# Four transfers instead of one for y and for x, spread between the loads of a weight ring

## What is computed

```
x  = attention(q, k, v, mem_k, mem_v)            # 3072 x 512, chunks of 32 with a small context
h  = x @ w_in;   g = elu(h);                     y = g @ w_out        # layer one
h2 = y @ w_in2;  g2 = s * relu(h2)**2 + b;       out = g2 @ w_out2    # layer two
```

## Time and profile before

| | |
|---|---|
| time, median of three runs | 1216.26 us (1216.18 to 1216.88) |
| profiled execution | 1211.64 us |
| its span, first to last instruction | 1209.9 us |
| mean granted TensorE clock | 0.975 of full |
| transfers in the span | 302.80 MB, mean 250 GB/s |

### The profile page before, as it was taken

One profiled execution on the slowest core, in us unless ns is written; L12 is line 12 of the kernel. 1 busy time (PEld: TensorE's weight loads), 2 busy tenths in 40 slices (PEclk: granted clock), 3 DMA queues, 4 the chain that ended last, 5 costly groups with the idle time before them and its releaser, 6 DMA issues.

```text
span 1209.9 us, 18083 instructions
## 1 busy us (share of the span) xinstructions
PE 1116.7 (92%) x5787; PEld 880.7 (73%) x5787; DVE 845.4 (70%) x1246; ACT 757.0 (63%) x1775; POOL 425.8 (35%) x458
## 2 busy tenths in 40 slices
PE   8993998988899899989899898899999999999998
PEld 4662776766677778767687676677787887887876
DVE  5773478448966965896848966948938559567385
ACT  4864687567656857747647557657566476566463
POOL 5789369743231322134334265672001010000000
PEclk9986999999999999999999999999999999999999
DMA  9994999999788888859997599887587666786664
GB/s 213 270 270 150 292 334 312 315 306 301 228 280 219 257 248 262 265 188 349 303 288 226 165 352 396 299 311 231 177 233 259 196 193 175 198 225 189 192 189 157
DMA packets 203750, 302.80 MB, mean 250 GB/s; under 512 B 112520, under 2 KB 120712, under 8 KB 203656
## 3 DMA queue, kind: packets, MB, share of 16 engines
q1 hardware_dynamic: 203656, 301.65, 81.8%
HBM read 226.10 MB, written 75.50 MB: 249 GB/s over the span
## 4 chain that ended last, share of the span: by engine, by line
PE 55%; DVE 12%; DMA 6%; issue 5%; ACT 5%; POOL 4%; SPq 0%; ACTq 0%; DVEq 0%; POOLq 0%
PE ps L1004 28%; PE ps L989 23%; DMA w_ring<-w_scratch 3%; DVE g_lo L1442 2%; DVE X L1354 2%; ACT ps L1084 2%; DVE xc_lo L1347 1%; DVE T L1437 1%; DVE X L1437 1%; POOL w_new L774 1%; PE ps L903 1%; DVE X L1411 1%; PE ps L955 1%; POOL att L774 1%; ACT elu L1163 1%
## 5 line engine op out<-in xcount | busy, mean ns | idle before, releaser
L989 PE MATMUL ps<-xc_hi,w_ring 128*128 128x512 f32 x1344 | 438.3, 398 | 24.2 <-issue 9.8
L1004 PE MATMUL ps<-g_hi,w_ring 128*128 128x512 f32 x1344 | 423.6, 396 | 26.9 <-issue 15.9
L989 PEld LDWEIGHTS ps<-xc_hi,w_ring 128*128 128x128 f32 x1344 | 254.9, 190 | 84.0 <-issue 13.6
L1004 PEld LDWEIGHTS ps<-g_hi,w_ring 128*128 128x128 f32 x1344 | 248.2, 189 | 92.6 <-issue 28.2
L989 PE MATMUL ps<-xc_lo,w_ring 128*128 128x512 f32 x672 | 263.9, 393 | 0.0
L1004 PE MATMUL ps<-g_lo,w_ring 128*128 128x512 f32 x672 | 263.3, 392 | 0.0
L774 POOL TENSOR_TENSOR w_new<-w_raw,w_new 128x256 fp32r<-128x256 f32 x182 | 167.0, 921 | 207.6 <-ACT w_new L1216 204.2
L1442 DVE TENSOR_TENSOR g_lo<-X,g_hi 128x512 fp32r<-128x512 f32 x240 | 187.9, 789 | 45.5 <-ACT g_hi L1202 45.0
L1202 ACT ACTIVATE g_hi<-X 128x512 fp32r<-128x512 f32 x240 | 149.2, 628 | 80.2 <-PE ps L1004 76.8
L1354 DVE TENSOR_TENSOR X<-s,ps 128x512 f32<-128x512 f32 x144 | 96.3, 682 | 108.7 <-ACT s L1144 80.7
L1004 PEld LDWEIGHTS ps<-g_lo,w_ring 128*128 128x128 f32 x672 | 126.9, 189 | 27.5
(11 more groups left out here) (115 smaller groups left out, 1343.2 us busy)
## 6 DMA issues: line engine op xcount, KB each, us to landing
w_ring<-w_scratch SPq DMA_DIRECT2D x336, 512.0 KB, 4.3
w_scratch<-w_new SPq DMA_DIRECT2D x182, 256.0 KB, 5.0
w_scratch<-att SPq DMA_DIRECT2D x42, 256.0 KB, 5.1
w_raw<-in_moe_w_in SPq DMA_DIRECT2D x16, 512.0 KB, 5.7
w_raw<-in_moe_w_out SPq DMA_DIRECT2D x16, 512.0 KB, 6.0
x_scratch<-y SPq DMA_DIRECT2D x3, 2048.0 KB, 9.8
att<-x_scratch SPq DMA_DIRECT2D x6, 1024.0 KB, 8.3
out<-elu SPq DMA_DIRECT2D x24, 256.0 KB, 4.4
```

The costliest lines, as they stand in the source:

```text
L989: last = nc.tensor.matmul(bank_of(st.pi, st.i), w[:, a, cols], x[:, st.pi, kk, :], start=(st.pi in (P1, P5, P4) and kk == 0 and n == 0), s ...
L1004: last = nc.tensor.matmul(bank_of(st.pi, d), w[:, a, cols], x[:, k % RING, :], start=(st.pi in (P1, P5, P4) and st.i == 0 and n == 0), sto ...
```

## The change

`save_y` stores one of the four blocks of y (512 KB) at each of s == 2, 4, 6 and 8. `load_x` loads one of the two blocks of a half of x (512 KB); for tiles 3 to 5 the four loads stand at s == 14, 18, 20 and 24, for tiles 1 and 2 the two loads of a half stand behind one another at the old step. Each of them stands behind the ring load of its step. The counts that the waits compare with are multiplied to fit.

```
         def wait_y_free(eng, t):
             if 0 < t <= TPL:
-                eng.wait_ge(y_saved, 16 * t)
+                eng.wait_ge(y_saved, 16 * KT * t)
...
-            def load_x(t, kk):
+            def load_x(t, kk, half):
...
-                    sp.wait_ge(y_saved, 16 * (i + 1))
+                    sp.wait_ge(y_saved, 16 * KT * (i + 1))
...
-                sp.dma_start(to.rearrange("p (k h) t -> p k (h t)", k=2),
-                             src[:, kk::2, i * TOK:(i + 1) * TOK]).then_inc(x_in[kk], 16)
-
-            def save_y(t):
+                sp.dma_start(to[:, 2 * half:2 * half + 2, :].rearrange("p h t -> p (h t)"),
+                             src[:, kk + 2 * half, i * TOK:(i + 1) * TOK]).then_inc(x_in[kk], 16)
+
+            def save_y(t, kt):
                 sp.wait_ge(y11_added, 2 * t + 2)
                 sp.wait_ge(c12_done, 2 * (6 * t + 5) + 2)
-                sp.dma_start(x1_dram[:, :, t * TOK:(t + 1) * TOK], y[:, :, :]).then_inc(y_saved, 16)
+                sp.dma_start(x1_dram[:, kt, t * TOK:(t + 1) * TOK], y[:, kt, :]).then_inc(y_saved, 16)
...
                 for kk in range(2):
-                    if t + 1 < TPL and s // 2 == LOAD_AT[kk] // 2 or TPL <= t + 1 < TILES and s == 14 + 2 * kk:
-                        load_x(t + 1, kk)
-                if t > 0 and s == 2 and t <= TPL:
-                    save_y(t - 1)
+                    for half in range(2):
+                        if t + 1 < TPL and s // 2 == LOAD_AT[kk] // 2 or TPL <= t + 1 < TILES and s == 14 + 6 * kk + 4 * half:
+                            load_x(t + 1, kk, half)
+                if 0 < t <= TPL and s % 2 == 0 and 2 <= s < 2 + 2 * KT:
+                    save_y(t - 1, s // 2 - 1)
...
-                pool.wait_ge(x_in[kk], 16 * t)
+                pool.wait_ge(x_in[kk], 32 * t)
...
-                act.wait_ge(x_in[kk], 16 * t)
+                act.wait_ge(x_in[kk], 32 * t)
```

## The result

| | before | changed |
|---|---|---|
| median | 1215.88 us (1212.52 to 1216.88, 6 runs) | 1204.07 us (1202.35 to 1206.23, 6 runs) |
| profiled execution, span | 1211.64, 1209.9 us | 1202.84, 1201.1 us |

The ratio is 0.991 (95% interval 0.9895 to 0.9924), that is 0.9% or 10.9 us less (the two medians lie 11.8 us apart). 6.8 were predicted, and the time lies 1.1 us under the range. The two profiled executions lie 8.8 us apart, and 2.1 of these do not come from the change: PE's first matmul with the weight ring starts at 117.86 in place of 119.95, and the first changed transfer, of the x of tile 1, is issued at 299.76. The other 6.7 us are close to the 6.8 that were predicted from this same profile of before.

A forecast was written before the change was run, and what follows sets the result against it. PE, 92% busy, was taken as the bound, losing time to ring loads queued behind y and x. Gains 3.8 + 2.9 + 0.7 - 0.6 = 6.8 us, taken from the median, gave 1209.5 us; range 1205.2 to 1214.6.

The forecast's parts named there:

- 3.28 us are lost in tile 2 and 7.12 us in tile 3: First up phases of 41.36 and 45.20 us, set against an unstopped one of 38.08 us, in one profile.
- 2.9 us for tile 2: Gain in tile 2's first up phase: its loss of 3.28 us goes down to between 0 and 1.0.
- 3.8 for tile 3: Gain in tile 3's first up phase from ring loads landing earlier; bounds 0 and 7.1 us.
- rival 3: All of it: up phases of tiles 2 and 3 fall to 38.1, 11.1 us won, 1205.2 us; chance 0.12.
- 0.7 predicted: Tile 4: the 0.70 us ring wait caused by tile 5's x goes, a gain of 0.7 us.
- 1.9 us behind x: Tile 3's first up phase: PE still held 1.9 us in all by s = 26, not 6 to 7.
- the signs: What would show the forecast right; in tile 3, the s = 18 load lands in 8 to 9 us, not 10.9.
- 0.6 us, on ACT: 700 to 760: ACT's lateness from waiting for saves, uncovered once PE's stop goes, costs 0.6 us; bounds 0 to 3.5.
- Rival 1: Full queue: saves take the places y and x leave in tile 3, nothing won there; 3.6 us, 1212.7; chance 0.17.
- Rival 2: Given back: PE waits in down phases paced by DVE and ACT; gain 0 to 2 us, 1215.3; 0.14 with rival 5.
- Rival 4: Slower: each transfer holds the queue a fixed time, 2.1 us; 17.7 us more in tiles 1 to 3, 1234; chance 0.05.
- Rival 5: Another transfer, not y or x, held the ring loads; no change to waits, 1216.3; 0.14 with rival 2.

The follow-up runs named there:

- the second timing: The changed kernel, unedited, timed and profiled again beside the kernel before in a later set: ratio 0.9926 (0.9901 to 0.9952).
- the fastest kernel: Against the changed kernel, y's four transfers moved to s = 2, 8, 14, 20 and x's to 30, 36, 42, 48: 0.9895 to the kernel before.
- before again: The kernel before, no edit, timed and profiled a second time: ratio 0.9995 (0.9982 to 1.0008).

## Why the prediction was wrong

**The step that failed** is the size of the loss: "3.28 us are lost in tile 2 and 7.12 us in tile 3", read from one profile and then taken from the median of other executions ("taken from the median 6.8 gives 1209.5"). Three more profiles of the same program have 3.2, 5.9 and 3.9 us more in the two up phases that the change acts on. On the means of the four the loss is 5.4 and 8.2 us, and the terms of the sum that were sized by it, 2.9 us for tile 2 and 3.8 for tile 3, come to 4.5 and 5.7. The loss itself is larger than in the first profile, and one profile gave no bound for that; with tile 4, 14.6 us could be won by the means, where rival 3 had 11.1.

**The mechanism**, fewer bytes ahead of a given ring load, was right for x and in tile 2; y in tile 3, at this spacing, won nothing (an up phase of 46.87 us with y alone in four, and of 41.01 with x alone against 41.02 with both). Against the first profile the terms come out close: tile 2 41.36 - 38.73 = 2.6 us (2.9 predicted), tile 3 45.20 - 41.02 = 4.2 (3.8 predicted), tile 4's up phase 42.91 - 41.92 = 1.0 (0.7 predicted). Against the means of the four profiles of before and the two of the changed kernel: tile 2 43.48 - 39.00 = 4.5, tile 3 46.32 - 40.61 = 5.7, tile 4 0.9; together 11.1.

That tile 3 came out close against the first profile is in part luck. No wait was priced behind y, and 1.9 us behind x; the trace has 0.52 and 0.78 us behind y, at the loads of s = 6 and 10, and none behind x (in the second profile 0.78 behind y and 0.15 behind x). The prediction says that from s = 10 on the same bytes stand ahead as before, but gives no price to PE's coming there sooner. Two of its numbers do not follow from its own sums: tile 3 gives 3.5 and 3.8 is taken, and the load of s = 18 would land 7.1 us after its issue, where the signs say 8 to 9; it was 6.9.

**What was given back** was foreseen at 0.6 us, on ACT. The first down phases of tile 3 and tile 4 are longer than before: 44.42 against a mean of 43.06, and 39.68 against 39.05, together 2.0 us. The sum 11.1 - 2.0 = 9.1 us lies at the edge of the interval of the timed gain (9.2 to 12.8 us) and at the gain of the second timing (0.9926, 9.0 us). The place was near, the engine was another. The wait for ACT that DVE had (3.55 us) is gone, as forecast; ACT's own waits for saves in 700 to 760 went only from 13.2 to 12.3 us. In the fastest kernel they are 6.3, and yet PE's wait stays at 2.5 to 2.6 us, with DVE at 93 to 97% of 740 to 760. So it is not the saves.

DVE's result is ready 0.10 us before PE goes on, in the changed kernel (755.21 and 755.31) as before (763.33 and 763.43); that DVE sets this wait is read from the traces and was not tried by giving DVE less work. By the same means the rest of the span nets to 0.1 us (the spans lie 9.0 us apart); in it the first down phase of tile 1 is 1.7 us longer (53.47 against 51.74), though no changed transfer is issued in it, and no run here gives the cause.

**The full queue** kept a part of the loss, as forecast in size though not in place: as long as y and x stand in the stretch where the queue has no gap, a stop stays. 1.9 us by s = 26 were forecast to be left of tile 3; 1.3 us of stops were, in an up phase 2.9 us longer than a free one. Wider spacing took the rest (38.13).

**The rivals.** Rival 1 (the full queue eats it) fell by the up phase of tile 3, though y alone did win nothing there. Rival 2 (given back) is real with 2.0 us, and too small. Rival 3 (all of it) was nearest in time, 1205.2, for another reason: not all of the loss went, but the loss was larger. Rival 4 (a fixed price for each transfer) fell by the kernel that splits in place: not slower. Rival 5 (y and x do nothing to the waits) fell by the ring waits, 8.1 us before and 1.8 after. The rule of the Trainium skill (DMA: Bandwidth & Descriptors, section Bandwidth) that larger transfers move faster did not decide here: with 512 KB where 2 MB and 1 MB stood the kernel was not slower in place and faster with distance.

## What to carry to other kernels

A large transfer in the queue of a just-in-time ring costs what it puts ahead of one ring load beyond that load's spare time; cut it, and set the pieces as far apart as their readers allow, since pieces that are close together in a full queue only move the stop. Waits for transfers in a nearly full queue differ from execution to execution, here by up to 5.9 us where the change is worth 9 to 11, and the total of one profile does not show whether it was a lucky one there, so a loss of that kind gets a wide upper bound or a second profile. An engine that waits for a stopped one shows its own lateness only when the stop is gone.

## What was not expected of the hardware

A 1 MB half of x was not always 2.55 us of queue. In tile 2 of the first profile the ring load of 562.44 landed in 3.7 us, at 566.1, and the half of x issued at 563.19 in 8.4, at 571.6: 5.5 us behind it. In the second profile of before ("before again") the same transfer came 6.6 us behind its ring load, and in the kernel split in place its two pieces came 2.8 and 2.1 us behind one another, 4.9 in all. In tile 3 of the first profile the halves took 2.9 and 2.5 us. While the slow half moved, the DMA moved less: 285 GB/s in 566 to 568 and 344 in 568 to 570 of the first profile, where 732 to 750 has 411. So the time that the prediction gives to 1 MB, 2.55 us, does not hold in tile 2. This is part of the scatter in tile 2, and would fit the gain of splitting in place; no run shows that it is the cause. Why a half takes so long just there was not found.

The stretches at a lower clock fall behind other gaps from execution to execution. In the first profile of before the gap of 1.86 us at 374.22 was followed by a granted clock of 0.66 in 375 to 380, and the gap of 2.54 at 403.30 by 1.00; in the changed kernel the same two waits were 1.87 and 2.52 us, and the clock fell to 0.72 (400 to 405) behind the second. Tile 1's phases differ by 1.4 to 1.5 us between the two profiles for it, up in the one and down in the other.
